# Own step lists for the first passes of a linear-attention and two-layer MoE kernel, with the weight loads, the first rotations and the masks moved

## The chip, the cores and the metric

One NeuronCore of a Trainium2 chip. Times are device microseconds of one launch. The kernel before took 1306.36 us, the median of 3 runs (1305.45 to 1306.60).

## The reference, cut to what matters

```
scale = min(mag, 0.999) / (mag + 1e-6)          # mag = |a_re + i a_im|, all (4, 8, 768, 48)
for t in range(768):                             # a complex decay per head and channel
    S = (a_re + i a_im)[t] * scale[t] * S + k[t] v[t]^T      # S: 48 x 48 per head
    y[t] = q[t] . Re(S)
x   = y as (3072 tokens, 384)
h   = silu(xn @ w_gate) * (xn @ w_val)           # xn: rms-normed x * rms_g; (384, 1536) weights
x   = h @ w_out                                  # (1536, 384)
e   = argmax over 8 experts of cosine(x, expert_emb) / tau
out = softmax weight * relu(x @ w1[e]) @ w2[e]   # (384, 1024), (1024, 384), top 1
```

## The kernel before

The first part of the kernel, up to about 950 us, does the recurrence, the gated layer (GLU) and the routing logits. The second part does the experts; the change leaves it alone.

The recurrence runs in 12 passes, each of U = 2 units of 128 time steps, all 8 heads at once. For a pass, four pieces of work belong together, named in the step lists by a stage:

- **sq** and **pre** prepare the decays. ScalarE squares a_re and a_im; VectorE adds them (m2, line 454), marks where a_re is negative (half, 457) and turns the sign of a_im there (459); ScalarE takes |a_re| (629) and scales half by -0.25 (631): this is the half-turn product. ScalarE takes the root (639); VectorE makes a1, den and rm (466 to 471, "sums"), GpSimd three products (373 to 378), VectorE the reciprocal (476), GpSimd two products (395, 399, "quotients"), ScalarE the arctangent (671) and a second copy of r (675, "double"). VectorE makes th (489); TensorE sums it over time in PSUM (778, 779), VectorE takes off whole turns (495, 500, "phase"). ScalarE takes sine and cosine (681 to 684) and GpSimd multiplies queries and keys by them, two products of 768 elements per unit (408, "rotate"). GpSimd's q k product (387) and VectorE's sum of it (483) are "own", the diagonal.
- **lev** turns r, q and k by TensorE (764), evacuated by ScalarE (601), in twelve blocks through two PSUM buffers ("turn"). Seven levels follow: TensorE multiplies blocks of keys and queries into pG (807, 801), and VectorE scales half of QT and KT (524, 526), copies pG into the attention matrix by a mask (528) and multiplies the decays pairwise (533). Then the keys are turned back (822), the outputs y gather in pM (838, 841), and the state products k v also go to pM (852), so that they wait until ScalarE has copied y out (702). VectorE decays the state and adds to it (539, 546).
- **glu** is one pass later: norm, scale, turn_in (860, 689, 558), then twelve gates (873 to 875: 18 matmuls each), each followed by a Silu on ScalarE (711) and hid on VectorE (572).
- **fin** is two passes later: w_out (887) in twelve "out" steps, route and logits.

Each engine walks through one list of steps, STEPS, in its order, and does what is its own; an engine starts nothing ahead of the list. `pipeline` (240) calls `body(i, stages)` for i = -2 to 13 and names the stages that take part. Pass -1 has a list of its own, FIRST_STEPS, which ends with the squares of pass 1. Bodies 0 and 1 use STEPS like the others. There are no "out" or "gate" steps to do in body 0 and no "out" in body 1; in their places TensorE runs `busy`, matmuls whose result is not used:

```
if "lev" in stages and "fin" not in stages and step in ("gate", "out"):
    busy(BUSY_TURNS if step == "out" else BUSY_LEVELS if x < 5 else BUSY_END)
```

The GLU weights are split into two float32r parts in body 0, between the levels ("wts", "split"): six pieces, each 128 rows by all 1536 columns of w_gate or w_val, one activation on ScalarE (694) and one operation on VectorE (563) each. They land in the two halves of hid, and SP loads the third only when the first is split (line 312). w_out is loaded ahead of them. SP loads the decays of the next pass once GpSimd has made tt (269).

GpSimd also builds the constants at the start: identity and triangle (335 to 343), zeros in A (348), the level masks by ten selections (353, 355), and eight copies of parts of them (359, 360).

Of the kernel before, what the change touches and what calls it, by code (L numbers as in the profile page):

```python
# [77 lines left out]
BUSY_TURNS, BUSY_LEVELS, BUSY_END = 2, 3, 1  # L78
# [12 lines left out]
    ("wts", "split", 0), ("lev", "level", 1), ("pre", "double", 0), ("pre", "double", 1), ("fin", "out", 9), ("fin", "out", 10),  # L91
    ("wts", "split", 1), ("lev", "level", 2), ("fin", "out", 11), ("fin", "square", 1), ("glu", "gate", 0),
    ("wts", "split", 2), ("lev", "level", 3), ("pre", "angle", 0), ("glu", "gate", 1),
    ("wts", "split", 3), ("lev", "level", 4), ("fin", "route", 0), ("pre", "angle", 1), ("glu", "gate", 2),
    ("wts", "split", 4), ("lev", "level", 5), ("pre", "phase", 0), ("glu", "gate", 3),
    ("wts", "split", 5), ("lev", "level", 6), ("pre", "phase", 1), ("pre", "own", 0), ("glu", "gate", 4),
    ("lev", "turn_back", 0), ("pre", "rotate", 0), ("pre", "own", 1), ("glu", "gate", 5), ("fin", "logits", 0),
    ("lev", "turn_back", 1), ("pre", "rotate", 1), ("glu", "gate", 6),
    ("lev", "output", 0), ("lev", "output", 1), ("glu", "gate", 7),
    ("lev", "state", 0), ("glu", "gate", 8), ("sq", "squares", 0), ("sq", "squares", 1), ("glu", "gate", 9),  # L100
    ("lev", "output", 2), ("lev", "output", 3), ("glu", "gate", 10), ("sq", "abs", 0), ("sq", "abs", 1), ("glu", "gate", 11),
# [6 lines left out]
    ("roots", 0), ("roots", 1), ("sums", 0), ("sums", 1), ("recip", 0), ("recip", 1),  # L108
    ("quotients", 0), ("tangent", 0), ("angle", 0), ("double", 0),
    ("quotients", 1), ("phase", 0), ("own", 0), ("tangent", 1), ("double", 1), ("angle", 1), ("phase", 1), ("own", 1),  # L110
    ("rotate", 0), ("rotate", 1))] + SQUARES
# [11 lines left out]
def steps_of(stages):  # L123
    return SQUARES if stages == ("sq",) else FIRST_STEPS if stages == ("pre", "sq") else STEPS


def build(nc, q, k, v, a_re, a_im, w_gate, w_val, w_out, rms_g, emb, tau, w1, w2, out, xd):
# [11 lines left out]
    with top:  # L139
# [19 lines left out]
        with a:  # L159
# [34 lines left out]
            emb_sb, embs = xn[0][0:NE, :], xn[1][0:NE, :]  # L194
# [7 lines left out]
            landing = [hid[:, i * NF // 2:(i + 1) * NF // 2, :].rearrange("p f t -> p (f t)") for i in range(2)]  # L202
# [24 lines left out]
            n_consts = n_first + 3 + 2 * LOW + 2 * NBLOCK  # L227

            def pview(u, ell):

# [1120 lines left out]
```

## Time and profile before

| | |
|---|---|
| median of 3 runs | 1306.36 us |
| the profiled execution | 1303.45 us, its span 1301.7 us |
| mean granted clock of TensorE | 0.981 of full speed |
| from the start to the first level operation of pass 0 | 60.3 us |
| one pass in the middle (257 to 328 us) | about 71 us |

The profile is of one execution. A stretch's row gives, for each engine, its busy time in it, so a row shows which engine is full. A timeline row gives start, duration, engine, line and operands; in brackets stands the idle time ahead of it and who ended it.

### The profile page before, as it was taken

How to read it: one execution, taken by the hardware profiler on the slowest of the kernel's cores; microseconds unless marked ns; L12 is line 12 of the kernel's file. 1: busy time of each engine (PE TensorE's matmuls, PEld its weight loads, DVE VectorE, ACT ScalarE, POOL GpSimd, SP SyncE). 2: the span in 40 equal slices, each digit the busy share in tenths (PEclk: the TensorE clock that was granted, in tenths of full speed). 3: DMA queues.
4: the chain of work that ended last, by engine and by line, in shares of the span. 5: the costliest groups of instructions: out<-in, count | busy, mean ns of one | idle time of the engine just before them, and what ended most of it. 6: DMA issues, size and time to landing. Idle time of an engine off the chain costs nothing. (4 is left out here: it accounts for less than half of the span.)

```text
span 1301.7 us, 46434 instructions
## 1 busy us (share of the span) xinstructions
PE 1203.5 (92%) x20081; PEld 1041.7 (80%) x20081; DVE 766.8 (59%) x1549; ACT 600.7 (46%) x1293; POOL 366.4 (28%) x361
## 2 busy tenths in 40 slices
PE   1788999999999999999999999999978999999996
PEld 0556787879687887878687887878857999999996
DVE  5696847485767658484667557263117555555553
ACT  3646354545546554646455554434222344333442
POOL 8506051323333150413333150200003122222221
PEclk9899999999999999999999999999997999999998
DMA  7142011111202020111111020000005634333410
GB/s 206 26 123 59 7 39 40 39 40 33 45 15 57 9 58 20 38 40 39 39 30 42 9 45 10 15 15 3 13 13 161 209 127 143 132 134 131 137 37 30
DMA packets 151845, 78.36 MB, mean 60 GB/s; under 512 B 130715, under 2 KB 144571, under 8 KB 151664
## 3 DMA queue, kind: packets, MB, share of 16 engines
q1 hardware_dynamic: 143264, 59.04, 17.0%
q0 software_dynamic: 4384, 11.88, 3.1%
q10 hardware_dynamic: 4016, 4.73, 1.0%
q8 instruction: 149, 2.44, 0.8%
q14 instruction: 32, 0.26, 0.1%
HBM read 66.15 MB, written 11.06 MB: 59 GB/s over the span
## 5 line engine op out<-in xcount | busy, mean ns | idle before, releaser
L887 PE MATMUL pO<-wo_sb,hid 128*128 128x384 f32 x576 | 206.9, 496 | 4.0 <-issue 2.8
L572 DVE TENSOR_TENSOR hid<-silu,pGV 128x256 f32<-128x256 f32 x144 | 60.0, 417 | 177.2 <-ACT silu L711 177.2
L887 PEld LDWEIGHTS pO<-wo_sb,hid 128*128 128x128 f32 x576 | 102.6, 191 | 58.6 <-issue 5.2
L873 PE MATMUL pGV<-xT_hi,wg_hi 128*128 128x256 f32 x432 | 139.4, 323 | 6.1 <-DVE hid L572 6.1
L711 ACT ACTIVATE silu<-pGV 128x256 f32<-128x256 f32 x144 | 55.4, 385 | 181.1 <-PE pGV L875 178.9
L1198 ACT ACTIVATE h_hi<-pH 128x256 fp32r<-128x256 f32 x128 | 49.1, 385 | 164.9 <-PE pH L1143 164.9
L875 PE MATMUL pGV<-xT_hi,wg_lo 128*128 128x256 f32 x432 | 122.4, 283 | 1.0 <-issue 1.0
L874 PE MATMUL pGV<-xT_lo,wg_hi 128*128 128x256 f32 x432 | 122.0, 282 | 0.0
L873 PE MATMUL pGV<-xT_hi,wv_hi 128*128 128x256 f32 x432 | 121.5, 281 | 0.0
L874 PE MATMUL pGV<-xT_lo,wv_hi 128*128 128x256 f32 x432 | 121.5, 281 | 0.0
L875 PE MATMUL pGV<-xT_hi,wv_lo 128*128 128x256 f32 x432 | 121.2, 281 | 0.0
L387 POOL TENSOR_TENSOR qcs<-qin,kin 128x384 f32<-128x384 f32 x24 | 25.0, 1041 | 312.4 <-ACT A L662 312.4
L807 PEld LDWEIGHTS pG<-QT,KT 96*32 96x32 f32 x7680 | 77.1, 110 | 43.8 <-issue 37.4
L1141 PE MATMUL pH<-x_hi,w_hi 128*128 128x256 f32 x384 | 108.7, 283 | 2.9 <-DVE h_lo L1316 1.5
L1143 PE MATMUL pH<-x_hi,w_lo 128*128 128x256 f32 x384 | 108.6, 283 | 0.0
L1142 PE MATMUL pH<-x_lo,w_hi 128*128 128x256 f32 x384 | 108.6, 283 | 0.0
L807 PE MATMUL pG<-QT,KT 96*32 96x16 f32 x7680 | 85.3, 185 | 21.3 <-issue 10.6
L524 DVE TENSOR_TENSOR QT<-QT,PP 96x512 f32<-96x512 f32 x144 | 98.0, 681 | 8.8 <-PE pG L807 8.7
L526 DVE TENSOR_TENSOR KT<-KT,PP 96x512 f32<-96x512 f32 x144 | 98.0, 681 | 0.0
L873 PEld LDWEIGHTS pGV<-xT_hi,wg_hi 128*128 128x128 f32 x432 | 82.4, 191 | 13.7 <-DVE hid L572 7.4
L1157 PE MATMUL pOO<-w_hi,h_hi 128*128 128x384 f32 x256 | 87.0, 340 | 0.0
L874 PEld LDWEIGHTS pGV<-xT_lo,wg_hi 128*128 128x128 f32 x432 | 82.5, 191 | 4.3
(213 smaller groups left out, 3043.9 us busy)
## 6 DMA issues: line engine op xcount, KB each, us to landing
w_sb<-in_moe_w SPq DMA_DIRECT2D x18, 1536.0 KB, 10.5
re<-in_a_re SPq DMA_DIRECT2D x24, 192.0 KB, 2.9
im<-in_a_im SPq DMA_DIRECT2D x24, 192.0 KB, 3.7
qin<-in_q SPq DMA_DIRECT2D x24, 192.0 KB, 2.8
kin<-in_k SPq DMA_DIRECT2D x24, 192.0 KB, 3.6
vin<-in_v SPq DMA_DIRECT2D x24, 192.0 KB, 3.3
routed_rows<-x ACTq DMA_DIRECT2D x24, 192.0 KB, 2.0
wo_sb<-in_moe_w_out SPq DMA_DIRECT2D x1, 2304.0 KB, 9.5
```

Of the source, the lines that this page charges most:

```text
L524: w.tensor_tensor(qr, qr, pv[:, :, 0:1].to_broadcast([D2, H * nb, L]), ALU.mult).then_inc(q_level[u], 1)
L526: w.tensor_tensor(kl, kl, pv[:, :, 1:2].to_broadcast([D2, H * nb, L]), ALU.mult).then_inc(k_level[u], 1)
L572: w.tensor_tensor(hid[:, f, :], act_g[f % 2], pGV[f % 2][:, TOKS:2 * TOKS], ALU.mult).then_inc(sm["h_ready"], 1)
L807: ins = mm.matmul(pG[u][at, h * ODD:(h + 1) * ODD], KT[u][:, h, at], QT[u][:, h, at].rearrange("p (n two l) -> p n two l", two=2, l=L)[:, ...
L873: mm.matmul(to, hi, x_hi[:, kk, :], start=(kk == 0), stop=False)
L874: mm.matmul(to, hi, x_lo[:, kk, :], start=False, stop=False)
L875: ins = mm.matmul(to, lo, x_hi[:, kk, :], start=False, stop=(kk == KC - 1))
L887: ins = mm.matmul(pO[:, 0:HD], hid[:, f, s_ * P:(s_ + 1) * P], wo_sb[:, f, :], start=(f == 0), stop=(f == NF - 1))
L1141: m.matmul(pH[f % 3][:, 0:ROWS], hi, x_hi[:, kk, :], start=(kk == 0), stop=False)
L1142: m.matmul(pH[f % 3][:, 0:ROWS], hi, x_lo[:, kk, :], start=False, stop=False)
L1143: ins = m.matmul(pH[f % 3][:, 0:ROWS], lo, x_hi[:, kk, :], start=False, stop=(kk == KC - 1))
L1157: m.matmul(pO2[s_][:, 0:HD], h_hi[:, f, rows], hi, start=(f == 0), stop=False)
```

## The change

What it does, part by part:

- Bodies 0 and 1 get lists of their own, ZERO_STEPS and ONE_STEPS. The squares, signs and roots of pass 1 move from the end of body -1 and the start of body 0 to behind the turns of body 0, its sums, reciprocals and quotients to between its levels. In body 1 the same holds for pass 2. `busy` now runs only where a "warm" step stands: with 2 or 1 matmuls behind the levels of body 0, with 1 in the turns of body 1.
- The weight splits move from body 0 to body 1. Each piece is now all 384 rows by a third (512) of the columns, in three operations of 512 columns per engine. Pieces land in the three thirds of wo_sb; gates 0 to 3 need the first two pieces only. w_out is loaded after the last split.
- Bodies -1 and 0 rotate queries and keys on VectorE, the others on GpSimd as before.
- The product on half is gone in every pass: half holds 0.5 or 0, the sign is turned by (half - 0.25), and the arctangent takes scale -4. "signs" is a step of its own.
- The eight mask copies are on ScalarE. A is cleared by VectorE in body -1, carry and state by GpSimd. The work on expert_emb moves to the end of body 0.
- In every pass: the state products go to pG, in a step "products" right after the output of the unit, and no longer wait for y's copy; the square of y goes into x2; SP loads the decays once ima and |a_re| are there, and its loop is written out.

```
-BUSY_TURNS, BUSY_LEVELS, BUSY_END = 2, 3, 1
+WARM_TURNS, WARM_LEVELS = 1, 2
+THIRD = FF // 3
...
+FIRST_STEPS = [("pre", step, u) for step, u in (
+    ("roots", 0), ("roots", 1), ("masks", 0), ("signs", 0), ("sums", 0), ("signs", 1), ("sums", 1), ("recip", 0), ("recip", 1), ("clear", 0),
+    ("quotients", 0), ("quotients", 1), ("tangent", 0), ("double", 0), ("angle", 0), ("phase", 0), ("tangent", 1), ("double", 1), ("angle", 1),
+    ("own", 0), ("phase", 1), ("rotate", 0), ("own", 1), ("clear", 1), ("rotate", 1))]
+ZERO_STEPS = [
+    ("lev", "turn", 0), ("lev", "turn", 1), ("lev", "turn", 2), ("lev", "turn", 3), ("lev", "turn", 4), ("lev", "turn", 5), ("lev", "first", 0),
+    ("lev", "turn", 6), ("lev", "turn", 7), ("next", "squares", 0), ("lev", "turn", 8), ("lev", "turn", 9),
+    ("lev", "turn", 10), ("lev", "turn", 11), ("next", "signs", 0), ("lev", "first", 1),
+    ("lev", "level", 0), ("next", "squares", 1), ("next", "signs", 1), ("next", "abs", 0), ("next", "abs", 1), ("pre", "roots", 0), ("pre", "roots", 1), ("lev", "warm", WARM_LEVELS),
+    ("lev", "level", 1), ("pre", "sums", 0), ("lev", "warm", WARM_LEVELS),
+    ("lev", "level", 2), ("pre", "sums", 1), ("pre", "recip", 0), ("lev", "warm", WARM_LEVELS),
+    ("lev", "level", 3), ("pre", "quotients", 0), ("pre", "recip", 1), ("pre", "quotients", 1), ("pre", "tangent", 0), ("lev", "warm", WARM_LEVELS),
...
+    ("emb", "names", 0), ("lev", "output", 0), ("lev", "output", 1), ("lev", "products", 0), ("lev", "state", 0), ("pre", "rotate", 0), ("pre", "rotate", 1),
+    ("lev", "output", 2), ("lev", "output", 3), ("lev", "products", 1), ("emb", "names_turned", 0), ("lev", "state", 1),
+]
+ONE_STEPS = [
+    ("lev", "turn", 0), ("lev", "turn", 1), ("glu", "norm", 0), ("lev", "warm", WARM_TURNS), ("lev", "turn", 2), ("lev", "turn", 3),
+    ("lev", "turn", 4), ("lev", "turn", 5), ("wts", "split", 0), ("lev", "warm", WARM_TURNS),
...
+    ("lev", "turn", 10), ("lev", "turn", 11), ("lev", "first", 1), ("glu", "turn_in", 0), ("next", "squares", 0), ("next", "squares", 1), ("next", "signs", 0),
+    ("next", "abs", 0), ("next", "abs", 1),
+    ("lev", "level", 0), ("next", "signs", 1), ("pre", "roots", 0), ("pre", "roots", 1), ("glu", "gate", 0), ("glu", "gate", 1), ("pre", "sums", 0),
+    ("pre", "sums", 1), ("wts", "split", 2),
+    ("lev", "level", 1), ("glu", "gate", 2), ("pre", "recip", 0), ("wts", "split", 3),
+    ("lev", "level", 2), ("pre", "quotients", 0), ("glu", "gate", 3), ("pre", "recip", 1), ("pre", "quotients", 1),
+    ("lev", "level", 3), ("pre", "tangent", 0), ("pre", "tangent", 1), ("pre", "double", 0), ("pre", "double", 1), ("glu", "gate", 4), ("wts", "split", 4),
+    ("lev", "level", 4), ("pre", "angle", 0), ("pre", "angle", 1), ("glu", "gate", 5), ("wts", "split", 5),
+    ("lev", "level", 5), ("pre", "phase", 0), ("glu", "gate", 6),
+    ("lev", "level", 6), ("pre", "phase", 1), ("pre", "own", 0), ("glu", "gate", 7),
+    ("lev", "turn_back", 0), ("pre", "rotate", 0), ("pre", "own", 1), ("glu", "gate", 8),
...
+            landing = [wo_sb[:, i * NF // 3:(i + 1) * NF // 3, :].rearrange("p f d -> p (f d)").rearrange("p (k f) -> p k f", k=KC) for i in range(3)]
...
+                body(-1, ("pre",))
+                body(0, ("next", "sq", "pre", "lev", "wts", "emb"))
+                body(1, ("next", "sq", "pre", "lev", "glu", "wts"))
...
+                    def third(n):
+                        if n >= 3:
+                            sp.wait_ge(sm["wlo_ready"], n - 2)
+                        at = n // 2 * THIRD
+                        sp.dma_start(landing[n % 3], (w_gate, w_val)[n % 2][:, at:at + THIRD].rearrange("(k p) f -> p k f", p=P)).then_inc(staged[n % 3], 16)
...
-                                sp.wait_ge(sm["t_ready"], n0 - U + u + 1)
+                                sp.wait_ge(sm["ima_ready"], (i - 1) * U + u + 1)
+                                sp.wait_ge(sm["absre_ready"], (i - 1) * U + u + 1)
...
-                                s.activation(half[u][:, :, :], half[u][:, :, :], ACT.Copy, scale=-0.25).then_inc(sm["half_ready"], 1)
...
-                                    s.activation(at[u][:, :, :], tt[u][:, :, :], ACT.Arctan).then_inc(sm["at_ready"], 1)
+                                    s.activation(at[u][:, :, :], tt[u][:, :, :], ACT.Arctan, scale=-4.0).then_inc(sm["at_ready"], 1)
...
-                                pe.wait_ge(sm["x_ready"], n0 + u + 1 + ONE)
+                                pe.wait_ge(v_loaded[u], (i + 1) * 16)
+                                pe.wait_ge(a_high[u], (i + 1) * A_COPIES + ONE)
...
-                                        ins = mm.matmul(pM[at, h * D:(h + 1) * D], KTM[u][:, h, at], v_t[u][:, h, :], start=True, stop=True)
+                                        ins = mm.matmul(pG[u][at, h * D:(h + 1) * D], KTM[u][:, h, at], v_t[u][:, h, :], start=True, stop=True)
...
+                                if m == 0 and f % (NF // 3) == 0:
+                                    pe.wait_ge(sm["wlo_ready"], 2 * (f * 3 // NF + 1))
```

## Rows read from the trace of the kernel before

**Rows 1.** The page, part 1.
```profile
PE 1203.5 (92%) x20081; PEld 1041.7 (80%) x20081; DVE 766.8 (59%) x1549; ACT 600.7 (46%) x1293; POOL 366.4 (28%) x361
```

**Rows 2.** Stretches: us, busy PE, PEld, DVE, ACT, POOL, PEclk, DMA share, GB/s.
```profile
60.00:98.00 38.00, 33.15 (x778) 21.92 (x769) 36.19 (x64) 18.41 (x28) 2.83 (x2) 0.96 0.37 106
98.00:130.00 32.00, 28.34 (x580) 20.04 (x579) 21.41 (x29) 21.91 (x44) 20.23 (x16) 0.95 0.30 59
130.00:161.00 31.00, 29.62 (x730) 24.37 (x729) 26.80 (x63) 10.92 (x25) 2.01 (x2) 1.00 0.04 9
...
257.00:328.00 71.00, 69.10 (x1485) 58.27 (x1484) 47.24 (x98) 38.36 (x85) 22.47 (x18) 1.00 0.17 36
```

**Rows 3.** What TensorE waited for, 260 to 616 us: total, times, longest.
```profile
PE pG L807 <- DVE qcs L528: 4.2, 10, 0.8
...
PE pGV L873 <- DVE hid L572: 2.6, 5, 0.6
```

**Rows 4.** Timeline, start to first level, then the last level: start, us, engine, line.
```profile
5.49 1.96 POOL L348 MEMSET A<- 128x1024 f32 x2
...
12.97 0.24 POOL L359 COPY level_mask<-x 32x80 f32<-32x80 f32 x1
...
16.48 0.99 POOL L373 TENSOR_TENSOR scratch<-sqre,rr 128x384 f32<-128x384 f32 x1
...
38.95 2.00 POOL L408 TENSOR_TENSOR cs<-cs,kin 128x768 f32<-128x768 f32 x1
...
45.80 1.06 ACT L601 ACTIVATE RK<-pT 96x512 f32<-96x512 f32 x2
...
60.34 0.69 DVE L524 TENSOR_TENSOR QT<-QT,RK 96x512 f32<-96x512 f32 x1 [2.22 <-PE pG L807]
...
97.33 0.16 DVE L533 TENSOR_TENSOR PP<-PP 96x8 f32<-96x8 f32 x1
```

**Rows 5.** Timeline, between the levels of pass 0 and pass 2.
```profile
97.66 1.28 ACT L681 ACT_TABLE_LOAD   x1
...
103.61 0.19 ACT L706 ACTIVATION_READ_ACCUMULATOR mag<-rows 128x1 f32 x1
...
115.49 1.06 ACT L601 ACTIVATE RK<-pT 96x512 f32<-96x512 f32 x2
...
129.64 0.68 DVE L524 TENSOR_TENSOR QT<-QT,RK 96x512 f32<-96x512 f32 x1
...
160.59 0.74 PEld L822 LDWEIGHTS pT<-ident,KT 96*128 96x128 f32 x8
...
168.53 0.55 DVE L483 TENSOR_REDUCE diag<-qcs 128x8 f32<-128x384 f32 x1 [6.58 <-POOL qcs L387]
...
183.82 0.42 DVE L572 TENSOR_TENSOR hid<-silu,pGV 128x256 f32<-128x256 f32 x1 [1.63 <-ACT silu L711]
...
185.75 0.36 DVE L466 TENSOR_SCALAR sqre<-mag 128x384 f32<-128x384 f32 x1 [0.25 <-ACT mag L639]
```

**Rows 6.** VectorE groups by line: 60 to 99, 34 to 60, 0 to 34 us.
```profile
L563 DVE SCALAR_TENSOR_TENSOR wv_lo<-hid,gcol,wv_hi 128x1536 fp32r<-128x1536 f32 x3 | 5.4, 1811 | 0.5 <-ACT wv_hi L694 0.5
...
L476 DVE RECIPROCAL scratch<-scratch 128x384 f32<-128x384 f32 x2 | 5.1, 2542 | 0.0
...
L467 DVE SCALAR_TENSOR_TENSOR rr<-scratch,mag 128x384 f32<-128x384 f32 x2 | 1.2, 578 | 0.0
```

**Rows 7.** Timeline, GpSimd and VectorE at once, twice.
```profile
89.73 1.83 POOL L387 TENSOR_TENSOR qcs<-qin,kin 128x384 f32<-128x384 f32 x1 [30.76 <-ACT A L662]
...
90.60 0.99 DVE L533 TENSOR_TENSOR PP<-PP 96x16 f32<-96x16 f32 x1
...
118.76 1.35 DVE L467 SCALAR_TENSOR_TENSOR rr<-scratch,mag 128x384 f32<-128x384 f32 x1
```

**Rows 8.** Two stretches with the clock lowered, columns as in rows 2.
```profile
632.00:636.00 4.00, 2.33 (x6) 1.10 (x5) 4.00 (x9) 2.92 (x5) 0.00 (x0) 0.81 0.21 41
636.00:640.00 4.00, 4.00 (x134) 2.53 (x133) 1.00 (x3) 0.00 (x0) 0.00 (x0) 0.76 0.00 0
```

More of the change, by code:

```diff
@@ new lines @@
+ONE_STEPS = [
+    ("lev", "turn", 0), ("lev", "turn", 1), ("glu", "norm", 0), ("lev", "warm", WARM_TURNS), ("lev", "turn", 2), ("lev", "turn", 3),
+    ("lev", "turn", 4), ("lev", "turn", 5), ("wts", "split", 0), ("lev", "warm", WARM_TURNS),
+    ("lev", "turn", 6), ("lev", "turn", 7), ("glu", "scale", 0), ("lev", "first", 0), ("lev", "warm", WARM_TURNS),
+    ("lev", "turn", 8), ("lev", "turn", 9), ("wts", "split", 1), ("lev", "warm", WARM_TURNS),
+    ("lev", "turn", 10), ("lev", "turn", 11), ("lev", "first", 1), ("glu", "turn_in", 0), ("next", "squares", 0), ("next", "squares", 1), ("next", "signs", 0),
[9 more added lines that the diff above has]
+    ("lev", "turn_back", 0), ("pre", "rotate", 0), ("pre", "own", 1), ("glu", "gate", 8),
+    ("lev", "turn_back", 1), ("pre", "rotate", 1), ("lev", "output", 0), ("lev", "output", 1), ("lev", "products", 0), ("glu", "gate", 9),
+    ("lev", "state", 0), ("sq", "squares", 0), ("sq", "squares", 1), ("sq", "signs", 0), ("sq", "signs", 1), ("glu", "gate", 10),
+    ("lev", "output", 2), ("lev", "output", 3), ("lev", "products", 1), ("sq", "abs", 0), ("sq", "abs", 1), ("glu", "gate", 11),
+    ("lev", "state", 1),
+]
@@ L226, in build @@
             n_first = 9
[L227 removed]
+            n_consts = n_first + 1 + 2 * LOW
             def pview(u, ell):
@@ L262, in load, with decays @@
                                      ).then_inc(loaded[u], 16)
[L264 to L265 removed]
+                    def decays(i):
                         for u in range(U):
[L267 to L272 removed]
@@ new lines, in _ @@
+                    decays(0)
+                    queries_and_keys(0)
+                    third(0)
+                    third(1)
+                    decays(1)
+                    values(0)
+                    third(2)
+                    queries_and_keys(1)
+                    decays(2)
+                    third(3)
+                    third(4)
+                    queries_and_keys(2)
+                    values(1)
+                    third(5)
+                    decays(3)
+                    sp.wait_ge(sm["wlo_ready"], 2 * KC)
@@ L319, in _ @@
+                    sp.dma_start(wo_sb[:, :, :], w_out.rearrange("(f p) d -> p f d", p=P)).then_inc(sm["wo_loaded"], 16)
+                    for i in range(2, NP):
+                        if 2 < i < NP - 1:
+                            decays(i + 1)
+                        if i < NP - 1:
+                            queries_and_keys(i + 1)
+                        values(i)
                 @block.gpsimd
@@ L344, in _ @@
                     assert step == n_first
+                    g.memset(carry[:, :, :], 0.0).then_inc(sm["carry_ready"], 1)
+                    g.memset(state[:, :, :], 0.0).then_inc(sm["state_ready"], 1)
                     done(g.memset(wide_mask[:, :, :], 1.0))
-                    for u in range(U):
-                        done(g.memset(A[u][:, :, :], 0.0))
                     for ell in range(LOW):
```

238 lines of the change are left out of this document (114 added, 124 removed).

## The prediction

> **What bounds the kernel now.** Read the page's busy times first [rows 1]: TensorE is busy 92% of the span, VectorE 59%. That alone says that an edit to VectorE or GpSimd is worth nothing. The busy times by stretch say where it isn't so [rows 2]. From pass 2 on, here 257 to 328 us, TensorE works 69.1 of 71 us and VectorE 47.2. The little that TensorE waits there, from 260 to 616 us, is for the level operations of VectorE, 4.2 us in ten times, and for hid, 2.6 us [rows 3]: under 2 us a pass, and none of it is for GpSimd, for the state update or for a load. Before pass 2 it is another kernel. From 60 to 98 us, the levels of pass 0, VectorE is busy 36.2 of 38 us and sets the pace, while much of TensorE's 33.2 us is the filler of busy(). From 130 to 161 us, the levels of pass 1, TensorE is busy 29.6 of 31 us with real gate work and VectorE 26.8. Between these lie stretches that wait on chains: the first 34 us, and 98 to 130 us, where VectorE has 21.4 us of work in 32.
>
> So the change can win only ahead of 186 us, and I cut that into five stretches by marks: A, up to the first level operation of pass 0 at 60.3 us; B, its seven levels, to 97.3 us [rows 4]; C, to the first level of pass 1 at 129.6 us; D, its levels, to the first turn back at 160.6 us; E, to the first sum for pass 2 at 185.7 us [rows 5]. Before, they last 60.3, 37.0, 32.3, 31.0 and 25.2 us.
>
> **The change, stretch by stretch.** *A.* GpSimd begins its sums at 16.5 us, right after the last mask copy, though their input is ready sooner [rows 4]. The change takes eight copies (from 13.0 us on, 3.4 us) and the two memsets of A (1.96 us) from GpSimd [rows 4] and gives it two of 384 columns, by the length of A's some 0.8 us. 4.6 us come free, but then VectorE's own sums and reciprocals, 2.54 us each [rows 6], come to the front, and one more table load may fall due on ScalarE, so I take 3 us. The first rotations take GpSimd up to 2.0 us per product of 768 elements, and the last keys are there at 41 us [rows 4]. On VectorE a level product of 512 elements takes 0.69 us [rows 4], so one of 768 about 0.95. But they wait behind phase 1 in VectorE's list, so I expect the last keys at 38 us. The larger part is an order: the first turned block is there when the keys are and is evacuated only at 45.8 [rows 4], because ScalarE first does the squares, signs and roots of pass 1. Own lists put those behind the turns. Turns from 34 us, twelve in 10 us behind keys at 38, put the first level at 44.3: A loses **16.0**.
>
> *B.* VectorE loses six weight splits of 1.81 us [rows 6], 10.9 us. It gets what A no longer does for pass 1: one half of the squares and both halves of the signs, minus those already done, 1.3; two sums of three operations of about 0.5 us, 2.8; two reciprocals, 5.0. Together 9.1. That would make 35.2 us. The third term is new: GpSimd's ten products for pass 1 now run beside VectorE's level operations and no longer beside waiting. Twice the trace shows what this costs [rows 7]: at 90.6 us a product of 16 elements, some 0.17 us otherwise, takes 0.99 while a GpSimd product runs, and at 118.8 us an operation of 0.58 us [rows 6] takes 1.35. Each product can so cost VectorE between 0 and about 0.95 us; a reciprocal beside it kept its 2.54 us [rows 6], so not all are paid. Of seven exposed ones I take half, 3 us, and 1 us for TensorE's answer between levels. B is 39.2, **+2.2**.
>
> *C.* Before, the first block of pass 1 was evacuated at 115.5 us, 18.2 after B [rows 5]: the state waited for y to leave pM and for GpSimd's rotations. With the products in pG and the rotations on VectorE what is left is ScalarE's list: y of the first half (some 3.4 us after B), then a table load, two groups of sines, y's copy and its square, which took it from 97.7 to 103.8 us before [rows 5], 6.1 us, and y's second copy and square, 1.0. So the first block of pass 1 goes at 10.5. From there to level 0 it took 14.2 us before (115.5 to 129.6). I add 0.8 for the norm, which now waits for VectorE's rotations; 1.6 for two splits on ScalarE, each about as long as VectorE's 1.8 but partly in its idle time; and 2.5 for the squares and signs of pass 2, three operations of 0.5 us on VectorE behind ScalarE's four, which now stand ahead of level 0. C is 29.6, **-2.7**.
>
> *D.* Here the bill comes. VectorE now has, inside the levels, four splits (7.4), two reciprocals (5.0), two sums (2.8), one half of signs (0.8), and four hid more (1.3): 17.3 us. Of its 26.8 [rows 2] some 24.2 are left once overlaps and the part after the turn back are taken off: 41.5 us. To it come GpSimd's ten products, between 0 and 9.5 us; half again, 5; and 1.2 us in which split 4 waits for ScalarE, which has two tangents, two doubles and a table load ahead of it. D is 47.7, **+16.7**. TensorE had five gates in its 29.6 us, with eight it has some 36, and lies below. Neither third 3 nor third 4 should be late: their loads are released by splits 0 and 1 in the turns, more than 10 us ahead.
>
> *E.* Three gates (5, 6, 7) have moved into D. A gate is 2.05 us, by the last hid at 183.8 us: 0.42 and 1.63 of waiting for the next [rows 5]. The rest stays: VectorE waits for the second half's diagonal until GpSimd is through with its rotation, as at 168.5 us [rows 5]. E is 18.9, **-6.3**.
>
> *The rest.* The half-turn product is 1.0 us of ScalarE per pass. ScalarE is busy 38.4 of 71 us [rows 2] and TensorE's waits name it nowhere [rows 3], so I cost it at nothing; its cover is TensorE's list of gates. The same holds for the state products in pG, for the square of xs into x2, and for the earlier loads of the decays: the DMA engines are 0.17 busy there [rows 2]. The load of w_out now comes last. It is released by split 5 near the end of D and is needed in pass 2, E's 19 us later. The sum is -16.0 + 2.2 - 2.7 + 16.7 - 6.3 = **-6.1 us**. The profiled execution took 1303.45 us around a span of 1301.7; against it the sum gives 1297.4, and against the median of the three runs, 1306.36, it gives **1300.3**.
>
> **The rule against it.** The two rows [rows 7] leave open whether every product of GpSimd is paid. The Trainium skill, SBUF — State Buffer, "Who interferes with whom", says that a VectorE instruction with two SBUF inputs and a GpSimd instruction that reads SBUF exclude each other for a whole instruction. By that rule the 3 and 5 us above stand at their upper bounds, and the sum would be +1.9 us and not -6.1, before anything that follows from it.
>
> **The rivals.** *Full blocking.* Each exposed GpSimd product costs VectorE its 0.95 us: 6.5 us in B for 3, and 9.5 in D for 5, so 8 us more, and the change ends at +1.9; GpSimd's own ten products wait as well, its quotients come later, and so do tangents and split 4, for which I add 2 to 3 us. That makes 1306.4 + 4.4 = **1310.8**. For it speaks that both rows show nearly the full length; against it, that at 89.7 us it was GpSimd that waited (1.83 us for a product of 1.0). It decides once blocking in B and D together passes 14 us. *No net change.* A lesser form, with 6 to 8 us lost to late loads, cold TensorE in the turns of pass 0, where the warming blocks are gone, or idle time in C: **1306**. *The other passes gain too.* If ScalarE's 1.0 us a pass or the earlier state did matter in the ten passes from 2 on, at up to 0.9 us each, this would bring 9 us: **1291**. The waits [rows 3] speak against it; but a shorter C is as easily underrated by 6 us as overrated, and gives the same time.
>
> Beside these, TensorE's program has another length. In the trace it stopped for 1.7 us for no wait that is shown, at 632 us, and the clock was then granted at 0.81 and 0.76 in two stretches of 4 us [rows 8]: 1.7 us and another 1.7, so about 3.4 us for such a stop. There are three such stops from 616 to 840 us, and this is the first; one more or less widens the range by 3 us either way.
>
> **How the numbers follow.** A gain near the sum, 1296 to 1303.6, has 0.33. The larger gain has 0.18, no net change 0.20, full blocking with what follows 0.29. A measurement tells this kernel from no change at about 0.2%, 2.6 us. So faster 0.51, same 0.20, slower 0.29. The range takes the larger gain with one stop fewer, 1288, and full blocking with a little more, 1312; on either side about one in ten is left.
>
> **What would show it.** In the profile after: the first level at 42 to 46 us and the second block of levels from 113 to 118 us (if the latter is above 120, B or C was mis-sized); D at 45 to 52 us, with VectorE busy above 0.9 of it and TensorE for once below 0.85; pass 2 beginning at 177 to 183 us. Level operations of VectorE that take 1.2 to 1.6 us beside GpSimd, more than eight in D, would show the full blocking. Passes 2 to 9 should keep their 71 to 72 us; if they shorten by over 0.5 us each, I was wrong to cost the steady edits at nothing. A wait of VectorE for wg_hi over 2 us would show late thirds.

## The result: slower by 1.0%, outside the range, and the profile after

The kernel after took 1318.46 us, the median of 4 runs (1314.68 to 1321.64), beside 1305.90 us for before in the same comparison (4 runs, 1301.35 to 1306.60). The ratio is 1.0102, 95% interval 1.0063 to 1.0142. The forecast was 1300.3 us in 1288 to 1312. The profiled execution of after took 1316.3 us, its span 1314.6, which is 12.9 more than before's. Where these are depends on four marks. Timeline of after, start, duration, engine and line: the first level operation of pass 0, the last, the first of pass 1, its first turn back, and the first sum of body 2.

```profile
44.19 0.69 DVE L572 TENSOR_TENSOR QT<-QT,RK 96x512 f32<-96x512 f32 x1 [0.59 <-PE pG L863]
85.92 0.15 DVE L581 TENSOR_TENSOR PP<-PP 96x8 f32<-96x8 f32 x1
113.94 0.68 DVE L572 TENSOR_TENSOR QT<-QT,RK 96x512 f32<-96x512 f32 x1
168.81 0.49 PEld L878 LDWEIGHTS pT<-ident,KT 96*128 96x128 f32 x5
187.93 0.36 DVE L513 TENSOR_SCALAR sqre<-mag 128x384 f32<-128x384 f32 x1 [0.25 <-ACT mag L694]
```

They answer to [rows 4, 5] and give the stretches:

| stretch | before | after | change forecast | change measured |
|---|---|---|---|---|
| A, to the first level | 60.3 | 44.2 | -16.0 | -16.1 |
| B, levels of pass 0 | 37.0 | 41.7 | +2.2 | +4.7 |
| C, to the levels of pass 1 | 32.3 | 28.0 | -2.7 | -4.3 |
| D, levels of pass 1 | 31.0 | 54.9 | +16.7 | +23.9 |
| E, to the first sum of body 2 | 25.2 | 19.1 | -6.3 | -6.1 |
| the rest | 1116.0 | 1126.7 | 0 | +10.7 |

(The prediction calls E's end the first sum for pass 2; it is that of body 2, which prepares pass 3. The mark is the same in both.) Stretches of after, columns as in [rows 2]:

```profile
44.00:86.00 42.00, 29.11 (x724) 18.45 (x712) 40.58 (x67) 14.09 (x29) 17.34 (x14) 0.76 0.11 21
86.00:114.00 28.00, 19.60 (x571) 15.82 (x572) 17.12 (x35) 23.50 (x47) 0.00 (x0) 1.00 0.18 52
114.00:169.00 55.00, 35.65 (x746) 32.38 (x745) 52.72 (x88) 22.17 (x42) 17.59 (x12) 0.75 0.37 99
257.00:328.00 71.00, 67.87 (x1475) 56.97 (x1474) 47.22 (x97) 36.81 (x80) 22.86 (x18) 1.00 0.17 36
```

In D VectorE is busy 52.7 of 55 us and TensorE 35.7: VectorE sets the pace. In C it is busy only 17.1 of 28. That is the first thing to see: the work that fills D would have had room just ahead of it.

The rest splits by three more marks, taken from each timeline: the first level operation of pass 2, the last hid, and the first transposed expert tile (pXX). I call the three stretches "steady", "routing" and "expert"; the last has the same code in both kernels.

| | levels of pass 2 begin | steady | routing | expert |
|---|---|---|---|---|
| before | 200.6 | 751.7 | 51.2 | 298.3 |
| after | 202.2 | 757.1 | 50.5 | 304.7 |

Of the 12.9 us, 1.6 are there when pass 2's levels begin, 5.4 come in the steady stretch and 6.5 in the expert part; the routing gives 0.7 back.

### The profile page after: what moved, and what is told of

Same layout as the page of the kernel before. It is cut to its first block and busy times, and to the rows that moved or that the text cites. A ratio compares the mean times of both kernels' runs of the same rounds, so it can differ in the third digit from the quotient of the medians.

```text
span 1314.6 us, 46105 instructions
## 1 busy us (share of the span) xinstructions
PE 1178.3 (90%) x19969; PEld 1029.0 (78%) x19969; DVE 786.6 (60%) x1569; ACT 595.6 (45%) x1291; POOL 358.1 (27%) x345
## 5 line engine op out<-in xcount | busy, mean ns | idle before, releaser
L863 PEld LDWEIGHTS pG<-QT,KT 96*32 96x32 f32 x7680 | 81.0, 113 | 62.8 <-issue 50.9
L934 PE MATMUL pGV<-xT_lo,wg_hi 128*128 128x256 f32 x432 | 122.9, 285 | 3.0 <-issue 3.0
L863 PE MATMUL pG<-QT,KT 96*32 96x16 f32 x7680 | 90.4, 187 | 39.0 <-DVE qcs L576 33.0
L935 PE MATMUL pGV<-xT_hi,wv_lo 128*128 128x256 f32 x432 | 122.8, 284 | 1.6 <-issue 1.6
L935 PE MATMUL pGV<-xT_hi,wg_lo 128*128 128x256 f32 x432 | 123.1, 285 | 0.0
L934 PE MATMUL pGV<-xT_lo,wv_hi 128*128 128x256 f32 x432 | 122.9, 285 | 0.0
L572 DVE TENSOR_TENSOR QT<-QT,PP 96x512 f32<-96x512 f32 x144 | 101.3, 703 | 5.6 <-PE pG L863 5.3
L574 DVE TENSOR_TENSOR KT<-KT,PP 96x512 f32<-96x512 f32 x144 | 102.0, 708 | 0.0
L934 PEld LDWEIGHTS pGV<-xT_lo,wg_hi 128*128 128x128 f32 x432 | 83.4, 193 | 5.2 <-issue 1.1
L1376 DVE SCALAR_TENSOR_TENSOR h_lo<-pH,h_hi 128x256 fp32r<-128x256 f32 x128 | 53.9, 422 | 55.5 <-ACT h_hi L1258 55.5
```

The lines of the kernel that those rows point to most:

```text
L572: w.tensor_tensor(qr, qr, pv[:, :, 0:1].to_broadcast([D2, H * nb, L]), ALU.mult).then_inc(q_level[u], 1)
L574: w.tensor_tensor(kl, kl, pv[:, :, 1:2].to_broadcast([D2, H * nb, L]), ALU.mult).then_inc(k_level[u], 1)
L863: ins = mm.matmul(pG[u][at, h * ODD:(h + 1) * ODD], KT[u][:, h, at], QT[u][:, h, at].rearrange("p (n two l) -> p n two l", two=2, l=L)[:, ...
L934: mm.matmul(to, hi, x_lo[:, kk, :], start=False, stop=False)
L935: ins = mm.matmul(to, lo, x_hi[:, kk, :], start=False, stop=(kk == KC - 1))
```

## The experiments

Ratios are to before, with their 95% interval. First three theories: the head is lost to VectorE and GpSimd blocking each other (F) or in part only (H) or to a cold TensorE (L); the steady part to stops of TensorE that depend on the position in its program (P) or on the instructions (I).

**e1, e2: TensorE's program padded.** Both kernels, ahead of TensorE's first work:

```
+for _ in range(112):
+    mm.matmul(pO[:, 0:8], upto[:, :], ident[:, 0:8], start=True, stop=True)
```

> 

> Kernel after, with 112 matmuls of 8 columns ahead of TensorE's first work (it idles there until 24 us), so that its program has again the length that the fillers gave it before. All that is computed stays. Theory P (position): from pass 2 on TensorE stops at fixed places of its program for no wait that is shown, 10.5 us in 9 stops before and about 20 us in after, and which instructions are hit depends only on how many stand ahead of them. Then the stops move, their sum falls by 5 us or more, and the time falls from 1318 to about 1308 to 1312, while the start of pass 2 stays near 188 us. Theory I (the instructions themselves): the state products, now right behind the output, make a longer run of short matmuls that TensorE's supply cannot follow; then the stops stay at the products, near 20 us, and the time within 2 us of after.

> 

> Kernel before, with the same 112 matmuls of 8 columns ahead of TensorE's first work. All that is computed stays. Theory P: the stops (10.5 us in nine) move and their sum changes; as before sat low, the time rises by 3 to 8 us though nothing else is touched. Theory I: the stops keep their sum, and the time stays within 2 us of 1306. In either case the marks of the first passes should not move by more than 0.5 us.

Measured: 1344.49 us (1.0318, 1.0289 to 1.0348) and 1353.84 us (1.0373, 1.0329 to 1.0417). The padding cost its own time. The group of it in e2, by line, count, busy us, mean ns of one, idle time before:

```profile
L734 PE MATMUL pO<-ident,upto 128*128 128x8 f32 x224 | 48.0, 361 | 5.1 <-POOL upto L342 5.1
```

Each of the 112 stands as two matmuls there. They overlap, and together they keep TensorE busy for 48 us, 0.43 us for each of the 112, which do not fit into the idle time. The times tell nothing; behind the head the stretches can still be read: steady 755.5 us in e1 and 757.1 in e2, and the stops over 0.3 us summed 18.8 and 17.0 us, for 20.6 in after and 10.5 in before. So padding moved before's stops and added to them, which speaks for P, while it took little from after's, which speaks for I.

**e3: the state products late again.** Kernel after, in the steady list only:

```
-("lev", "output", 1), ("lev", "products", 0), ("glu", "gate", 7),
-("lev", "state", 0), ...
+("lev", "output", 1), ("glu", "gate", 7),
+("lev", "products", 0), ("lev", "state", 0), ...
```

> 

> Kernel after, with the step of the state products moved in the steady list only (pass 2 on) back to where the state step stands, behind the gate. They still go to pG. Theory I: four of the stops in after are at the products; with a gate between output and products they go, some 6 us, and the time falls to about 1312. Theory P: the number of instructions ahead of each place changes by 108 within a pass and not at all beyond; the stops land on a gate or a level instead, the sum stays near 20 us, and the time within 2 us of after.

Measured: 1311.25 us (1.0057, 1.0024 to 1.0090), some 7 less than after. By the ratios it is 0.45%, 5.9 us, and the two intervals overlap a little, so the traces have to carry the reading. The steady stretch took 749.6 us, for 757.1 in after and 751.7 in before. What TensorE waited for from 202 to 868 us for no reason that the profile shows; in after:

```profile
PE pG L910 <- issue: 6.5, 6, 1.6
PE pG L863 <- issue: 2.7, 4, 1.4
PE pT L960 <- issue: 2.6, 2, 1.5
PE pGV L934 <- issue: 1.9, 2, 1.1
PE pGV L935 <- issue: 1.6, 2, 0.9
PE pO L947 <- issue: 1.5, 2, 0.9
PE pM L895 <- issue: 0.3, 2, 0.2
```

and in e3:

```profile
PE pG L863 <- issue: 3.7, 5, 1.6
PE pT L960 <- issue: 2.6, 2, 1.3
PE pO L947 <- issue: 1.2, 2, 0.9
PE pM L895 <- issue: 1.1, 5, 0.3
PE pM L898 <- issue: 0.2, 1, 0.2
```

L910 is the products step. It stood in the waits of after with six stops and is gone in e3, and so are those at the gates (L934, L935). TensorE's busy time in the 738 us from 202 to 940, in before, after and e3:

```profile
202.00:940.00 738.00, 712.80 (x14844) 599.54 (x14843) 447.16 (x946) 369.12 (x808) 191.57 (x152) 0.99 0.13 29
```

```profile
202.00:940.00 738.00, 704.53 (x14792) 592.32 (x14780) 449.70 (x945) 362.53 (x792) 194.28 (x152) 1.00 0.13 29
```

```profile
202.00:940.00 738.00, 712.43 (x14914) 599.39 (x14910) 449.53 (x949) 364.14 (x795) 191.55 (x152) 1.00 0.13 29
```

It idles 25.2, 33.5 and 25.6 us: the place of the step costs 8 us of TensorE, and taking it back gives them back. That is what theory I said of the step; what it leaves to theory P is taken up with "The rest" below.

**e4: GpSimd's ten products on VectorE.** Kernel after, bodies 0 and 1, one of five per unit:

```
-g.tensor_tensor(dd[u][:, :, :], a1[u][:, :, :], den[u][:, :, :], ALU.mult)
+w.tensor_tensor(dd[u][:, :, :], a1[u][:, :, :], den[u][:, :, :], ALU.mult)
```

> 

> Kernel after, with GpSimd's ten products (sums and quotients) of bodies 0 and 1 each done by VectorE instead, in place; all that is computed stays. Each costs VectorE about 0.53 us more. Theory F (full blocking, every exposed GpSimd product costs VectorE its 0.95 us and GpSimd the same): 10 x 0.53 added and 9.5 taken away in D, 6.5 in B, plus the hand-overs: D falls by 4 us or more from 53, B by 1 to 2 from 41.7, pass 2 begins 5 us or more earlier than 187.9. Theory H (half of them, as I had forecast): added and taken away are equal in D (5.3 against 5), B gets 2 us longer, and pass 2 begins within 2 us of 187.9. Theory L (the loss of D is latency, VectorE waiting for a cold TensorE at a granted clock of 0.6 to 0.7 between levels): D grows by up to 5 us.

Measured: 1314.03 us (1.0072, 1.0036 to 1.0107). D took 51.6 us (114.4 to 166.1) for 54.9, B 41.5 for 41.7, and pass 2's levels began at 199.5, 2.7 earlier than in after. The time lies between F and H: F wanted 4 us or more in D, where 3.3 came, and 1 to 2 in B, where 0.2 came. The same operations in D, first in after, then in e4, where two of GpSimd's twelve operations are left:

```profile
L572 DVE TENSOR_TENSOR QT<-QT,PP 96x512 f32<-96x512 f32 x12 | 9.7, 807 | 0.0
L574 DVE TENSOR_TENSOR KT<-KT,PP 96x512 f32<-96x512 f32 x12 | 9.0, 746 | 0.0
L612 DVE SCALAR_TENSOR_TENSOR wg_lo<-wo_sb,gcol,wg_hi 128x512 fp32r<-128x512 f32 x6 | 6.4, 1112 | 1.4 <-ACT wg_hi L751 1.4
L523 DVE RECIPROCAL scratch<-scratch 128x384 f32<-128x384 f32 x2 | 5.1, 2540 | 0.0
L612 DVE SCALAR_TENSOR_TENSOR wv_lo<-wo_sb,gcol,wv_hi 128x512 fp32r<-128x512 f32 x6 | 4.8, 851 | 0.0
```

```profile
L590 DVE TENSOR_TENSOR KT<-KT,PP 96x512 f32<-96x512 f32 x12 | 8.2, 681 | 0.0
L588 DVE TENSOR_TENSOR QT<-QT,PP 96x512 f32<-96x512 f32 x12 | 8.2, 681 | 0.0
L539 DVE RECIPROCAL scratch<-scratch 128x384 f32<-128x384 f32 x2 | 5.1, 2543 | 0.0
L628 DVE SCALAR_TENSOR_TENSOR wg_lo<-wo_sb,gcol,wg_hi 128x512 fp32r<-128x512 f32 x6 | 4.1, 746 | 1.1 <-ACT wg_hi L767 1.1
L628 DVE SCALAR_TENSOR_TENSOR wv_lo<-wo_sb,gcol,wv_hi 128x512 fp32r<-128x512 f32 x6 | 4.1, 730 | 0.8 <-ACT wv_hi L767 0.8
```

The levels are 2.3 us longer in after (9.7 + 9.0 - 16.4), the splits 3.0 (11.2 - 8.2), the small decay products 1.4 and the sums 1.5, together 8.2 us for ten products of GpSimd. On VectorE the ten took 5.5 us, so 2.7 were to be gained, and 3.3 were. The level operations lasted as long in e4, with the clock at 0.80 in D, as in before at full clock, and VectorE never waited for TensorE in D: theory L falls.

**e5, e7: SP's loop.** Kernel before with the loop written out, and kernel after with it put back:

```
-with sp.Fori(1, B - 1) as b:
+for b in range(1, B - 1):
     batch(b, range(NJ), False)
```

> 

> Kernel before with one edit: SP's loop over the two middle batches is written out, as the change does. All that is computed stays. The expert part, whose code the change does not touch, took 298.2 us in before from its first transposed tile to the end and 303 to 306 in after and its variants, 4.9 us of which are a wait for the second set of expert weights, whose load lasts 10.5 us for 7.7 before. Theory L (the written-out loop gives SP and its queue another state, and that delays this load): the expert part gets 303 us or more and the time rises by about 5. Theory D (it is the number or shape of the DMA packets ahead of it, so the thirds): it stays at 298 and the time within 2 us of before.

> 

> Kernel after with SP's loop over the two middle batches put back, with the waits of after in it. All that is computed stays. Theory L: the expert part returns to 298 us, the time falls by about 5 from 1318. Theory D: the expert part stays at 303 or more and the time within 2 us of after.

Measured: 1306.07 us (0.9997, 0.9978 to 1.0015) and 1318.09 us (1.0086, 1.0066 to 1.0106). The expert part took 299.0 us in e5 and 301.3 in e7, where theory L wanted 303 and 298. So the loop written out did not lengthen it; the 301.3 of e7, in one profile, fit neither theory.

**e6: padding with waits.** Kernel before, `for _ in range(224): pe.wait_ge(consts, n_first)` behind TensorE's first transposes.

> 

> Kernel before with 224 semaphore waits that are satisfied at once, ahead of TensorE's filler and pass work and behind its first transposes, in the time in which TensorE idles (up to about 30 us): the padding of the runs before, which cost its own time there, now with instructions that should cost nothing. All that is computed stays. Theory P (position in the program): the marks up to pass 2 stay within 1 us, and from pass 2 to the last hid the stops move, with their sum 3 us or more away from 10.5 and the time up by 2 to 6 us. Theory I: the sum stays within 2 us of 10.5 and the time within 2 us of before.

Measured: 1307.88 us (1.0008, 0.9988 to 1.0027). The stops stood at other places and summed 14.3 us for 10.5, but pass 1's levels began 3.5 us later, so the head was not left alone. By the time it is no difference: the position moves single stops, and by itself does not explain what after lost. Inconclusive for more than that.

**e8: e3 and e4 together.**

> 

> Kernel after with both edits that helped alone: the state products behind the gate again from pass 2 on, and GpSimd's ten products of bodies 0 and 1 on VectorE. All that is computed stays. If the two are independent (one in the head, one in the steady passes), -7.2 and -4.4 us of the medians add: 1318.5 - 11.6 = 1307, with pass 2's levels beginning at 199.5 us and the stops at about 10 us. If the stops depend on the position in the program (theory P), the gain of the steady part is not tied to the edit and may be anything from 0 to 7 us: 1307 to 1314.

Measured: 1309.82 us (1.0017, 0.9997 to 1.0036); levels of pass 2 at 200.9, stops 11.0 us, expert part 304.5. The two gains add about as expected.

**e9, e10: both kernels once more.**

> 

> Kernel after once more, for a second profile. Theory K (the longer expert part belongs to the kernel): from the first transposed tile to the end it takes 303 to 306 us again, with a wait for the second expert weights of 4.5 us or more. Theory R (it falls anew with each execution): it can come out anywhere between 298 and 306, and the wait between 1 and 6 us. The stops of TensorE should be the same 20 or so at the same instructions, 20 us or more in sum, if they belong to the program.

> 

> Kernel before once more, for a second profile. Theory K: the expert part takes 298 us within 1. Theory R: anywhere between 298 and 306. The stops should be the same nine at the same instructions, about 10 us in sum, if they belong to the program.

Measured, one run each: 1322.56 and 1304.07 us. After's stops (those over 0.3 us, from 180 us on) came back at the same instructions, in sum 22.4 us for 20.6; before's 11.2 for 10.5. They belong to the program. The steady stretch took 761.8 us in after and 749.4 in before: with the first profiles, a mean loss of 8.9 us. The expert part took 303.3 and 300.9 us; it varies by about 3 within a kernel, so neither theory holds as put.

**e11: the preparation of pass 2 in the turns.** The kernel of e3, with the squares, signs and |a_re| of pass 2 moved to the end of body 0's list, and body 1's list changed:

```
 ONE_STEPS = [
-    ("lev", "turn", 0), ("lev", "turn", 1), ("glu", "norm", 0), ...
+    ("glu", "norm", 0), ("pre", "roots", 0), ("pre", "roots", 1), ("lev", "turn", 0), ("lev", "turn", 1), ...
+    ("pre", "sums", 0), ("pre", "sums", 1), ("lev", "turn", 4), ... ("pre", "recip", 0), ...
+    ("lev", "turn", 6), ("lev", "turn", 7), ("pre", "recip", 1), ("wts", "split", 0), ...
+    ("lev", "turn", 8), ("lev", "turn", 9), ("pre", "quotients", 0), ...
```

> 

> The kernel with the state products late (the run e3), with body 1's preparation of pass 2 moved: its squares, signs and |a_re| to the end of body 0, its roots, sums, reciprocals and quotients into the turns of body 1, where VectorE idles 11 of 28 us, as the steady list has them; the splits stay, two at the turns and four in the levels. All that is computed stays. Theory F (D was long for VectorE's own work and for GpSimd's products beside the levels): D loses two reciprocals, two sums, the signs (9.4 us) and some 8 us of blocking, and falls from 54 to about 38; C grows by 3 to 6; pass 2's levels begin at 192 to 196 us, and the time falls to 1302 to 1306. Theory M (the memory port is always paid): the products block in the turns as well; VectorE then has no room in C, which grows by 12 or more, and pass 2 begins within 3 us of 202.

Measured: 1305.51 us (1.0002, 0.9976 to 1.0027), 6 less than e3. C grew from 28.0 to 34.3 us (85.7 to 120.0), the levels of pass 1 fell to 41.7 us up to their last operation, for 54.2 in after, and pass 2's levels began at 197.5 for 202.3. Stretches of e11, C's end and D:

```profile
85.00:120.00 35.00, 22.15 (x559) 17.66 (x556) 29.02 (x46) 28.49 (x53) 11.52 (x10) 0.78 0.06 18
120.00:162.00 42.00, 33.30 (x745) 30.09 (x746) 36.72 (x77) 16.83 (x36) 3.46 (x2) 0.87 0.56 148
```

GpSimd's products (11.5 us) now lie in C, where VectorE has room. The gain is a little smaller than theory F said (38 us for the levels, and pass 2's from 192 to 196). As VectorE's own sums and reciprocals moved together with GpSimd's products, e11 does not tell what each of the two is worth; e4 prices the products alone.

**e12: before's weight loads in thirds. e13: spare loads.** The edits:

```
+for c in range(3):
+    at = slice(c * FF // 3, (c + 1) * FF // 3)
+    sp.dma_start(landing[n % 2][:, at], ...[..., at]).then_inc(staged[n % 2], 16)
-act.wait_ge(staged[x % 2], (x // 2 + 1) * 16)
+act.wait_ge(staged[x % 2], (x // 2 + 1) * 48)
```
```
+spare = sb(a, "spare", [P, 8])
+for c in range(8):
+    sp.dma_start(spare[:, c:c + 1], w_gate[0:P, c:c + 1], ...).then_inc(spare_loaded, 16)
```

> 

> Kernel before with one edit: each load of 128 rows of a gate weight is issued as three loads of 512 columns to the same place, so that SP's queue carries 18 loads with rows of 2 KB, as in after, and not 6 with rows of 6 KB. All that is computed stays. Theory D (the longer expert part comes from the number or shape of the packets that went before on this queue): the load of the second expert weights lasts 10 us or more for 7.1 to 9.4, the expert part 303 us or more for 298 to 301, and the time rises by 4. Otherwise this is not the cause: the expert part stays at 298 to 301 and the time within 2 us of before.

> 

> The kernel of the run e11 with eight spare loads of one column of 128 values each on SP's queue, in body 1, into a tile that nothing reads. All that is computed stays. Theory Q (the place in the queue's ring decides how the load of the second expert weights falls): it lasts another time than e11's 11.3 us, the expert part moves from 305 towards 299, and the time from 1305.5 to about 1300. Otherwise the expert part stays at 303 to 306 us, and the time within 2 us of e11's.

Measured: 1307.28 us (0.9992, 0.9967 to 1.0017), expert part 300.1; and 1297.95 us (0.9926, 0.9900 to 0.9952), expert part 303.3. Neither moved the expert part, yet e13 took 7.5 us less than e11.

**e14 to e18: what the spare tile does.** e14 and e15 are e11 and e13 again, e16 is e11 with the tile and its semaphore but no load, e17 is after with tile and loads, e18 is before with

```
 gcol = sb(a, "gcol", [P, KC])
+spare = sb(a, "spare", [P, 8])
+spare_loaded = sem("spare_loaded")
```

> 

> The kernel of the run e11 once more, on the same chip as the next three. Theory S (the eight spare loads themselves, or what they shift, gave the 7.5 us of e13): it takes again 7 us more than the next run. Theory C (chips differ, and e13 stood on another than e11): it lies within 2 us of the next run, at about 0.993 of before.

> 

> The kernel of the run e13 once more. Theory S and theory C both expect 0.993 of before if that run stood for the kernel; under theory C the run before this one has the same ratio, under theory S it has 1.000.

> 

> The kernel of e11 with the spare tile of 8 columns and its semaphore, and none of the eight loads: it moves the tiles behind it in SBUF by 32 bytes per partition and changes no instruction's work. Under theory S by the loads it takes what e11 takes; under theory S by the tiles' places it takes what e13 takes; under theory C all are equal.

> 

> Kernel after with the eight spare loads of one column. All that is computed stays. Under theory S it takes some 7 us less than after, 1.004 of before for 1.010. Under theory C it stays at 1.009 to 1.012 of before.

> 

> Kernel before with the spare tile of 8 columns and its semaphore, and nothing else. Before and after allocate the same tiles in the same order, so their places are equal. Theory T (the places of the tiles, or what comes with them, cost either kernel the same): before falls by about 8 us too, to 0.994 of itself, and the run e16 has beaten before only by that. Theory O (the effect belongs to the program of after's family): before stays within 2 us of 1305, and e16 is a better kernel by 7 us.

Measured:

| | us | ratio to before | interval |
|---|---|---|---|
| e14 | 1305.62 | 1.0007 | 0.9986 to 1.0027 |
| e15 | 1297.82 | 0.9957 | 0.9943 to 0.9972 |
| e16 | 1297.33 | 0.9946 | 0.9930 to 0.9963 |
| e17 | 1312.73 | 1.0053 | 1.0026 to 1.0079 |
| e18 | 1297.63 | 0.9941 | 0.9921 to 0.9960 |

The tile and its semaphore do it without a load, and they do the same for before. The edit moves the tiles behind gcol (the split of x, silu, hid) by 32 bytes per partition and adds a semaphore; which of the two acts was not tried apart. A trace of it is the pace of TensorE within a gate. The first and the last of the 18 matmuls of one gate, in before:

```profile
219.71 0.36 PE L873 MATMUL pGV<-xT_hi,wg_hi 128*128 128x256 f32 x1
221.82 0.28 PE L875 MATMUL pGV<-xT_hi,wv_lo 128*128 128x256 f32 x1
```

and in e18:

```profile
220.24 0.37 PE L875 MATMUL pGV<-xT_hi,wg_hi 128*128 128x256 f32 x1
222.32 0.28 PE L877 MATMUL pGV<-xT_hi,wv_lo 128*128 128x256 f32 x1
```

Over the gates from 205 to 850 us that TensorE runs without a pause, the median of this distance is 2.10 to 2.11 us in all fifteen profiles without the tile, and 2.05 to 2.09 us in the five with it. In e18 it is 0.02 us less than in before, which makes some 3 of the 9 us over 144 gates; in e16 it is 0.05 less, some 7 us. The mean durations of single matmuls do not show it: for the gate's second one it is 283 ns in before, 281 in its repeat e10 and 281 in e18. Why the tile or the semaphore changes the pace stays open.

## Why the prediction was wrong, step by step

**A was right**, -16.1 for -16.0. The first level came at 44.2, inside 42 to 46, and on the way that was forecast: the first turned block was evacuated at 34.8 us and the last keys were rotated at 38.9, for 34 and 38.

**B, +4.7 for +2.2.** The failing term is GpSimd's blocking, taken as 3 us. Level operations beside GpSimd took 1.48 us for 0.68, as these rows of VectorE and GpSimd at once show:

```profile
54.58 1.48 DVE L572 TENSOR_TENSOR QT<-QT,PP 96x512 f32<-96x512 f32 x1
55.98 1.48 DVE L574 TENSOR_TENSOR KT<-KT,PP 96x512 f32<-96x512 f32 x1
```
```profile
54.21 1.30 POOL L402 TENSOR_TENSOR scratch<-sqre,rr 128x384 f32<-128x384 f32 x1 [24.26 <-DVE rr L514]
55.66 1.26 POOL L405 TENSOR_TENSOR sqre<-sqre,im 128x384 f32<-128x384 f32 x1
56.88 1.44 POOL L407 TENSOR_TENSOR mag<-mag,rr 128x384 f32<-128x384 f32 x1
```

Over B the level operations and decay products are some 7 us longer than the same shapes without GpSimd: 5.7 of them go away with the ten products in e4, the rest stands beside GpSimd's four products of "own", which the sum did not count. The other terms were 1.5 us too high.

**C, -4.3 for -2.7**, 28.0 us for 29.6: a small term sized too high. The marks were right, the levels of pass 1 at 113.9. VectorE waited 4.0 and 2.4 us for ScalarE's halves of splits 0 and 1, which cost nothing there. By the forecast's last sign, a wait for wg_hi over 2 us, the thirds would have been late; they were not, as ScalarE waited for no load in C. The splits stood behind its evacuations.

**D, +23.9 for +16.7, is where the head was lost.** By its own terms: blocking 8.2 us for 5; VectorE's own operations 43.9 (busy 52.1 up to the last level operation, less 8.2) for 41.5; waits 2.2 for 1.2; and 0.6 from the last level operation to the turn back. That makes 54.9 for 47.7. The step that failed is "half again, 5": of the 9.5 us of the upper bound, 8.2 were paid. Next to it VectorE's own operations were sized 2.4 us too low. The forecast had said that more than eight level operations of 1.2 to 1.6 us would show it. Three of the 28 in D did, by which the full blocking would have been dismissed. That was a poor mark: more of the blocking fell on splits, sums and small decay products. The Trainium skill, SBUF — State Buffer, "Who interferes with whom", had been set against the sum: by that rule the head came out at +1.9 us. It was +2.2. The trace agrees with the rule in the size of the blocking, with e4 against after as the test (8.2 of 9.5 us in D, 5.7 of 6.5 in B). That the whole head agrees to 0.3 us is luck: D's other terms were 4.0 us too low and those of B and C together 3.1 too high. A reciprocal kept its 2.54 us beside GpSimd, as in [rows 6], but a one-input tensor_scalar of 0.35 us took 1.17:

```profile
119.61 0.35 DVE L513 TENSOR_SCALAR sqre<-mag 128x384 f32<-128x384 f32 x1
120.94 1.17 DVE L513 TENSOR_SCALAR sqre<-mag 128x384 f32<-128x384 f32 x1
120.57 1.32 POOL L402 TENSOR_TENSOR scratch<-sqre,rr 128x384 f32<-128x384 f32 x1 [36.40 <-DVE rr L514]
```

The sentence that I had drawn on is about two SBUF inputs; the same section of the Trainium skill says that tensor_scalar can contend as well, in a mode with two ports, and this row fits that.

**E was right**, -6.1 for -6.3.

**"The rest" was costed at nothing and cost 10.7 us.** This is the larger error: 5.4 us of it lie in the steady stretch (8.9 by the mean of two profiles each) and 6.5 in the expert part, while the routing and the way to pass 2's levels give some back. The step that failed is "so I cost it at nothing", which the prediction then extends: "The same holds for the state products in pG". The prediction said of them that the waits name them nowhere, and so it asked only what the products had waited for, not what stands ahead of them on TensorE. Output and products are now one run of short matmuls with no gate between; TensorE stopped there six times for up to 1.6 us, and again in each profile of a kernel with that order (up to 2.3 us in e17), and e3 takes 8 us of idle time away by moving the step alone. The forecast had seen such stops in before [rows 8], counted three from 616 to 840 us where its trace has four of 1.2 to 1.7 us, and widened the range by 3 us for one more or less; it took them for an accident of the program's length.

The traces also show what TensorE waits for there. A DMA queue of the kind "instruction" brings packets of 16 KB, one for each 256 of TensorE's instructions (weight loads and waits counted). Of 256 stops over 0.3 us between 180 us and the last hid, in all twenty profiles, 250 stand at the same place of such a block, its 194th or 195th instruction when blocks are counted from the first one recorded, and each of these ends 1.1 to 1.7 us after a packet of that queue was through. Here is one of them in after; the last row is the queue's in the DMA view from 688 to 689.4 us, with one packet, which ran from 688.1 to 689.2:

```profile
688.42 0.59 PE L910 MATMUL pG<-vin,RK 128*32 128x48 f32 x28
690.47 0.33 PE L910 MATMUL pG<-vin,RK 128*32 128x48 f32 x10 [1.47 <-issue]
q8 instruction: 1, 0.02, 5.1%
```

What fits all of these is that TensorE waits for the next 256 instructions of its program; no run changed that supply itself. Both theories then have their part. Position (P) sets where a block begins: a pass is some 11.8 blocks long, so the places come back after five passes, 59 blocks (325.6 and 690.5 us, 388.5 and 753.7, in after), and the padding of e2 and e6 moved them. The instructions (I) set whether the block is late: of the stretches from one such place to the next that TensorE ran through in under 3 us, three in four ended in a stop over 0.3 us; of those that took over 4 us, one in 36. In after, six of the places fall among the products, with nothing but short matmuls for the 256 instructions ahead (1.7 to 1.8 us). In e3 the same six have a gate's long matmuls ahead, four of them take 4.5 to 5.1 us, and none has a stop over 0.3 us.

**The expert part** took 4.7 us more on average: 297.6 to 301.3 us in seven profiles of before and its variants, 301.3 to 305.9 in thirteen of after and its variants. In after ScalarE waits long for the second expert weights, issued at 1010.29:

```profile
1020.82 0.63 ACT L1241 ACTIVATE w_hi<-w_sb 128x512 fp32r<-128x512 f32 x1 [5.93 <-DMA w_sb<-in_moe_w]
```

In before they are issued at 1003.42:

```profile
1011.12 0.63 ACT L1181 ACTIVATE w_hi<-w_sb 128x512 fp32r<-128x512 f32 x1 [2.60 <-DMA w_sb<-in_moe_w]
```

10.5 us for 7.7. SP's loop written out, loads in thirds, spare loads and the tiles' places did not move it (299.0, 300.1, 303.3 and, with the tile, 298.9 in before and 305.0 in e16); the cause stays open.

**The rivals.** Full blocking, forecast at 1310.8 with a chance of 0.29, was the true mechanism of the head (+2.2, where it put +4.4); the slower side was underrated because the head was taken for the whole. Its own mark, blocking in B and D together past 14 us, lies in between: 13.9 us for the twenty products alone, 15.3 with those of "own". The clock, granted at 0.75 in D, cost nothing that VectorE waited for there.

**A version that beats both?** e16 takes 0.9946 of before, by e3's and e11's orders and the tile. But before with the tile takes 0.9941 (e18), so the new order as a whole shows no gain: A's 16 us are spent again in the other stretches of the head, and in the expert part. What remains is that one spare tile made before faster by 0.6%.

## What to carry to other kernels

When work is moved from a stretch that waits into one that is full, price it with every engine that shares the data's memory: here each 384-column product of GpSimd beside VectorE cost VectorE 0.8 us, and moving it, with VectorE's own preparation, to where VectorE idles gave 6 us (e11). A step that is moved for its wait also changes what its engine runs back to back; look at both neighbours of its new place, and keep some long matmuls between runs of short ones. Before a small gain is credited to an order, put a spare tile into both kernels: here it moved either by 0.6%.

## What the runs showed that I had not expected

- A spare tile of 32 bytes per partition, with a semaphore, took 8 us (0.6%) off either kernel with no step changed (e14 and e16 on one chip, and e18).
- Most of TensorE's stops come back at the same instructions in each execution of a program: 20 and 23 of them over 0.3 us in after's two profiles, nine and ten in before's. They stand at one place of each 256 instructions, where the next 16 KB of the program have only just come, and their sum goes from 10 to 21 us with the place of one step.
- A padding of 112 f32 matmuls of 8 columns took 48 us of TensorE (e2): for a filler the number of columns is not the price.
